# A sliding-window mix and an ELU MLP on one core: another prologue before the first token block

## The reference

```python
# x (4, 4096, 192), weight_gen (4, 4096, 8, 7), w_in (192, 2048), w_out (2048, 192), all float32
w = exp(weight_gen - max over the 7 taps);  w = w / (sum over the taps + 1e-9)
x_pad = x with 6 zero tokens in front of each sequence
mixed[b, s, h, :] = sum over k of w[b, s, h, k] * x_pad[b, s + k, h, :]     # 8 heads of 24 channels
h = mixed.reshape(16384, 192) @ w_in
g = where(h > 0, h, exp(min(h, 0)) - 1)
out = g @ w_out
```

## Time and profile before

| what | us |
|---|---|
| median of 3 runs (1242.32 to 1243.68) | 1242.58 |
| the profiled execution's own time | 1241.61 |
| its span | 1239.8 |
| TensorE busy | 1203.3 |
| ScalarE busy | 968.9 |
| VectorE busy | 822.3 |
| GpSimd busy | 705.1 |

### The profile page before, as it was taken

How to read it: one execution, slowest core, us unless ns; L and a number is a source line. 1 busy time by engine, 2 the same in 40 slices (tenths; PEclk the granted TensorE clock), 3 DMA queues, 4 the chain that set the end, 5 groups by cost and what they waited for, 6 DMA issues and landing times.

```text
span 1239.8 us, 19812 instructions
## 1 busy us (share of the span) xinstructions
PE 1203.3 (97%) x6848; PEld 1088.5 (88%) x6848; DVE 822.3 (66%) x1453; ACT 968.9 (78%) x1897; POOL 705.1 (57%) x298
## 2 busy tenths in 40 slices
PE   2699999999999999999999999999999999999998
PEld 1699999999999999999999999999999999999998
DVE  7866666666666666666666666666666666666665
ACT  3588787888788788787787787887887887888786
POOL 8677654567545576554576555576554676555600
PEclk9899999999999999999999999999999999999999
DMA  7011011111011110011110111110111110110000
GB/s 228 33 49 35 15 50 48 48 49 34 14 48 49 48 48 23 26 48 49 48 48 14 35 48 48 49 48 3 46 49 48 48 49 0 48 49 13 13 13 13
DMA packets 17086, 51.82 MB, mean 42 GB/s; under 512 B 1944, under 2 KB 8212, under 8 KB 17040
## 3 DMA queue, kind: packets, MB, share of 16 engines
q1 hardware_dynamic: 17040, 51.36, 12.5%
HBM read 38.77 MB, written 12.58 MB: 41 GB/s over the span
## 4 chain that ended last, share of the span: by engine, by line
PE 96%; DVE 3%; ACT 0%; DMA 0%; SPq 0%; POOL 0%; issue 0%; DVEq 0%; POOLq 0%
PE slot L599 48%; PE acc L605 29%; PE acc L609 17%; DVE wout L509 1%; PE slot L587 1%; PE slot L589 1%; DVE prod L477 0%; DVE prod L481 0%; DMA xwin<-in_x_dram 0%; SPq L248 0%; DVE prod L485 0%; DVE slot L554 0%; DVE g_lo L560 0%; DVE prod L487 0%; POOL xwin L293 0%
## 5 line engine op out<-in xcount | busy, mean ns | idle before, releaser
L554 DVE SCALAR_TENSOR_TENSOR slot<-em,slot 128x512 f32<-128x512 f32 x512 | 356.3, 696 | 388.2 <-ACT em L437 386.5
L605 PE MATMUL acc<-wout,g_hi 128*128 128x384 f32 x2048 | 468.2, 342 | 9.5 <-DVE g_lo L560 9.5
L431 ACT ACTIVATE em<-slot 128x512 f32<-128x512 f32 x512 | 305.0, 596 | 194.1 <-PE slot L599 194.1
L605 PEld LDWEIGHTS acc<-wout,g_hi 128*128 128x128 f32 x2048 | 369.2, 188 | 46.5 <-issue 9.9
L560 DVE TENSOR_TENSOR g_lo<-slot,g_hi 128x512 fp32r<-128x512 f32 x511 | 349.9, 685 | 1.9
L437 ACT ACTIVATE em<-em 128x512 f32<-128x512 f32 x512 | 323.5, 632 | 16.4
L609 PE MATMUL acc<-wout,g_lo 128*128 128x192 f32 x2048 | 326.7, 266 | 0.2 <-DVE g_lo L560 0.2
L609 PEld LDWEIGHTS acc<-wout,g_lo 128*128 128x128 f32 x2048 | 311.8, 190 | 3.0 <-DVE g_lo L560 0.5
L337 POOL TENSOR_TENSOR prod<-xwin,probs 128x5376 f32<-128x5376 f32 (+1 forms) x32 | 308.2, 9631 | 8.1 <-POOL probs L323 6.5
L444 ACT ACTIVATE g_hi<-slot 128x512 fp32r<-128x512 f32 x511 | 298.3, 584 | 13.1 <-DVE slot L554 11.6
L599 PE MATMUL slot<-xt,win_hi 128*128 128x512 f32 x512 | 214.6, 419 | 2.7 <-DVE xt L522 2.7
(11 more groups left out here) (47 smaller groups left out, 586.0 us busy)
## 6 DMA issues: line engine op xcount, KB each, us to landing
xwin<-in_x_dram SPq DMA_DIRECT2D x30, 960.0 KB, 4.8
out_dram<-outs SPq DMA_DIRECT2D x32, 384.0 KB, 2.4
wg<-in_weight_gen_dram SPq DMA_DIRECT2D x32, 112.0 KB, 2.3
wout_raw<-in_moe_w_out_dram SPq DMA_DIRECT2D x4, 384.0 KB, 9.0
win_raw<-in_moe_w_in_dram SPq DMA_DIRECT2D x1, 768.0 KB, 6.2
win_rest_raw<-in_moe_w_in_dram SPq DMA_DIRECT2D x2, 384.0 KB, 8.2
xwin<-in_x_dram SPq DMA_DIRECT2D x1, 768.0 KB, 10.5
xwin<-in_x_dram SPq DMA_DIRECT2D x1, 384.0 KB, 4.1
```

The costliest lines, as they stand in the source:

```text
L431: nc.scalar.activation(em[:, i % 2, :], slot[s][:], ACT.Exp).then_inc(s_exp, 1)
L554: nc.vector.scalar_tensor_tensor(out=slot[s][:], in0=em[:, i % 2, :], scalar=0.0, in1=slot[s][:], op0=ALU.min, op1=ALU.max).then_inc(s_g, 1)
L605: pe.matmul(acc[j][:, 0:2 * d_model], g_hi[:, f % GBUFS, chunk(j)], wout[:, f, :], start=(f == 0), stop=False)
```

## The change

- **Joint softmax.** The weights of blocks 0 and 1 are loaded first, and one softmax over both (64 rows of 7 per partition) runs on VectorE and ScalarE; GpSimd only scales.
- **The mix of block 0.** VectorE takes tiles 0 and 1 (before: 0 to 2). Its scaled weights go to a PSUM slot, the products of taps 0 to 3 to the four accumulator banks, those of taps 4 to 6 to SBUF, and each sum takes one input from PSUM. GpSimd takes tiles 2 and 3.
- **Part loads.** Four of the eight of window 0 are issued by ScalarE's queue.
- **Weights.** w_in comes in four quarters, like w_out. For the first two quarters of w_in and the first of w_out ScalarE writes the high half a second time, into PSUM (`mirror`), and VectorE's low half is the raw value in SBUF minus that copy. The low halves of all other quarters are GpSimd's: three after the products of block 1's mix, three after its pair sums, one after its last sums. Their high halves are ScalarE's, at chunks 0, 1, 2, 4, 5, 6 and 8 of block 0.
- **First chunks in halves.** Tiles 0 and 1 are transposed first, and the first three first products run over their 256 tokens; then the same for tiles 2 and 3.
- **Softmax of block 2** stands at chunks 5, 8, 9 and 12 of block 0 (7, 10, 11 and 12 before).

```diff
-            sp.dma_start(wg[:, 0, :], wg_v[:, 0:TILES, :]).then_inc(s_wg[0], 16)
+            for n in range(2):
+                sp.dma_start(wg[:, n, :], wg_v[:, n * TILES:(n + 1) * TILES, :]).then_inc(s_wg[n], 16)
             sp.dma_start(xwin[:, 0, halo:, :], x_v[:, 0:TILES, :]).then_inc(s_x[0], 16)
...
+            sp.wait_ge(s_zero, 1)
+            for at in range(0, P // 2, parts_per_batch):
+                reach_back(sp, 0, at)
...
+            load_win(0)
+            load_win(1)
+            load_wout(0)
             sp.dma_start(xwin[:, 1, halo - TILES:, :], x_v[:, 0:2 * TILES, :]).then_inc(s_x[1], 16)
+            sp.wait_ge(s_zero, 2)
+            for at in range(0, P, parts_per_batch):
+                reach_back(sp, 1, at)
+            load_wout(1)
+            load_win(2)
+            load_wout(2)
+            load_win(3)
+            load_wout(3)
...
@@ GpSimd, from block 1's mix on @@
+            pool.wait_ge(s_x[1], 16)
+            pool.wait_ge(s_reach[1], 16 * batch * len(REACH_PARTS))
+            pool.wait_ge(s_vmix, VMIX)
+            pool.wait_ge(s_add, ADDS)
+            products(1, 0, TILES // 2, last=False)
+            products(1, TILES // 2, TILES)
+            low_half("out", 1)
+            low_half("in", 2)
+            low_half("rest", 2)
+            pair_sums(one_)
+            shifted(two_)
+            low_half("out", 2)
+            low_half("in", 3)
+            low_half("rest", 3)
+            last_sums(one_)
+            guarded(two_)
+            low_half("out", 3)
...
@@ ScalarE @@
+            for kind, bank in (("in", slot[2][:]), ("rest", slot[3][:])):
+                hi_half(kind, 0)
+                mirror(kind, 0, bank)
+            hi_half("in", 1)
+            hi_half("rest", 1)
+            hi_of_pair(0, 0, 0, 1)
+            act.wait_ge(s_vmix, VMIX)
+            mirror("in", 1, acc[0])
+            mirror("rest", 1, acc[1])
+            hi_half("out", 0)
+            mirror("out", 0, wout_banks())
+            hi_of_pair(0, 1, 1, 2)
...
@@ VectorE, after its mix @@
+            low_half("in", 0, slot[2][:])
+            low_half("rest", 0, slot[3][:])
+            lo_of_pair(0, 0, 0, XPARTS)
+            low_half("in", 1, acc[0])
+            low_half("rest", 1, acc[1])
+            low_half("out", 0, wout_banks())
+            lo_of_pair(0, 1, 1, 2 * XPARTS)
...
@@ TensorE @@
             for k in range(X_STEPS):
-                if (k + 1) * PAIR > VECTOR_TILES:
+                if k == 1:
                     pe.wait_ge(s_add, ADDS)
                 transposes(0, k, k)
-            pe.wait_ge(s_wlo, 2)
-
-            pe.wait_ge(s_xlo, XPARTS * X_STEPS)
-            for f in range(LAG):
-                first_product(0, f, slot_of(0, f))
+                if k == 0:
+                    pe.wait_ge(s_wlo, 2)
+                pe.wait_ge(s_xhi, XPARTS * (k + 1))
+                for f in range(LAG):
+                    first_product(0, f, slot_of(0, f), slice(k * W, (k + 1) * W), filled=(k == 1),
+                                  when=XPARTS * (k + 1) if f == 0 else None)
```

More of the change, by code:

```diff
@@ L327, in body @@
[L327 to L338, removed]
+                r = slice(first_tile * heads, ROWS)
@@ new lines, in scaled, with products @@
+                nc.gpsimd.tensor_tensor(rows(probs[:, q, :])[:, r, :], rows(probs[:, q, :])[:, r, :],
+                                        spread(rec, kernel)[:, r, :], ALU.mult).then_inc(s_psoft, 1)
+            def products(q, first, end, last=True):
+                done = nc.gpsimd.tensor_tensor(prod_of(first, end), taps_of(q, first, end), weights_of(q, first, end),
+                                               ALU.mult)
+                if last:
+                    done.then_inc(s_prod, 1)
@@ L359, in softmax_vector @@
+            body(two_)
+            body(Block(1, 1))
+            with pool.Fori(2, BLOCKS // 2) as pair:
+                for parity in range(2):
+                    body(Block(pair, parity))
         def softmax_vector(b, step):
@@ new lines, in _, with spread @@
+            both_probs = probs[:].rearrange("p q (r k) -> p (q r) k", k=kernel)
+            def spread(t, k):
+                return t.unsqueeze(2).broadcast_to([P, t.shape[1], k])
+            for q in range(2):
+                dve.wait_ge(s_wg[q], 16)
+            nc.vector.tensor_reduce(first_max[:], both, AX.X, ALU.max).then_inc(s_vsoft, 2)
+            dve.wait_ge(s_vsoft, 2)
+            nc.vector.tensor_tensor(both_probs, both, spread(first_max[:], kernel), ALU.subtract).then_inc(s_psoft, 2)
@@ new lines, in _ @@
+            nc.vector.tensor_tensor(prod[:, BANK_TAPS:, 0:end].rearrange("p k (r g) -> p k r g", g=group),
+                                    taps_of(0, 0, VECTOR_TILES, (BANK_TAPS, kernel)), bank_weights((BANK_TAPS, kernel)),
+                                    ALU.mult).then_inc(s_vmix, 1)
+            dve.wait_ge(s_vmix, 3)
+            nc.vector.tensor_tensor(prod[:, BANK_TAPS:, 0:end], banks[:, 0:half, :], prod[:, BANK_TAPS:, 0:end],
+                                    ALU.add).then_inc(s_vmix, 1)
@@ new lines, in _ @@
+            total = banks[:, half, :]
+            for k in range(half - 1):
+                dve.wait_ge(s_vmix, 4 + k)
+                nc.vector.tensor_tensor(total, total, prod[:, BANK_TAPS + k, 0:end], ALU.add).then_inc(s_vmix, 1)
+            dve.wait_ge(s_vmix, 6)
+            total_t = total.rearrange("p (t d) -> p t d", d=d_model)
+            last_t = prod[:, kernel - 1, 0:end].rearrange("p (t d) -> p t d", d=d_model)
+            nc.vector.tensor_tensor(mixed[:, 0, 0:VECTOR_TILES, :], total_t[:, :, 0:P], last_t[:, :, 0:P],
+                                    ALU.add).then_inc(s_vmix, 1)
```

280 lines of the change are left out of this document (160 added, 120 removed).

## The result

The changed kernel takes **1231.61 us** (median of 4 runs, 1230.49 to 1233.91); the kernel before, run beside it, 1242.45 (1242.28 to 1243.68). The ratio is 0.991, 95% interval 0.9898 to 0.9923. The forecast was 1229.5 with a range of 1226 to 1235. The profiled execution is the fastest of the four: 1230.49 with a span of 1228.7, so its times are good for places and lengths, and 1.1 us too good for the total.

A forecast was written before the change was run, and what follows sets the result against it. Block 0's slow start, with VectorE and GpSimd taking turns, costs time beyond TensorE's pace. GpSimd's chain 48.95 + 18.04 = 67.0 against 80.10 gains 13.1; 1241.61 - 13.1 = 1228.5, plus 1.0 to the median: 1229.5 us, range 1226 to 1235.

The forecast's parts named there:

- Rival 1: Window loads come late because the two queues' issues take turns: 1.7 us more, 1231.2 us (1233 if worse); chance 0.14.
- Rival 2: TensorE's clock falls during its wait at block 1's transposes, costing 2.3 us: 1231.8 us; chance 0.16.
- The mark: The critical chain's entry when block 0 ends, 80.10 before; forecast at 67.0, a gain of 13.1 us.
- The start of the mixes: Block 0's prologue: joint softmax (3.4 us) done at 6.75, then GpSimd's scaling 0.35 and a turn of 0.25: 7.35.
- GpSimd's first tiles: GpSimd's mix of tiles 2 and 3 in block 0: 10.43 us plus 0.2 of fixed parts, ending at 18.0.
- Window 1: Block 1's token window, for which GpSimd would wait after its scaling, until 19.5 (bounds 17.5 and 21.6).
- Six low halves: GpSimd's low halves ahead of the last sums of block 1's mix: 3584 elements, 8.0 us.
- Transposes to mark: TensorE from the transposes of block 1's first two tiles to the end of block 0: 18.04 us.
- TensorE's own chain: Block 0: first exponential at 22.4, second products at 26.8, transposes reached at 45.3, 3.6 us ahead of GpSimd.
- one of the signs that the prediction named for being wrong: TensorE waiting elsewhere in block 0 (for g_lo or a weight), window 1 landing past 22, or block 1 waiting too.
- Rival 3: GpSimd isn't last in block 0; TensorE's chain ends it at 63.3, a gain of 16.8: 1225.8 us; chance 0.13.
- Rival 4: VectorE instructions with one PSUM input still keep GpSimd out: block 0 ends at 87.5, 1250 us; chance 0.03.

The follow-up runs named there:

- experiment 4: Two kernels: the change with all eight window 0 part loads on the sync queue, 1232.42 us; with early activation-table load and weights held until window 0 landed, 1232.28 us.
- window ahead of the weights: The changed kernel with the activation table loaded early and the loads of w_in and w_out held back until window 0 has landed: 1232.28 us.
- the early table: The changed kernel with a tiny exponential first on ScalarE to load the activation table, its tile allocated last so no other moves: 1229.62 us.
- all loads on sync: The changed kernel with all eight part loads of window 0 issued by the sync queue, as before the change: 1232.42 us.
- whole chunks: The changed kernel with block 0's first three chunks whole (512 tokens) after both pairs of tiles: 1231.92 us.
- the late copy: The changed kernel with ScalarE's copy of quarter 1 of w_out moved one chunk later: 1231.97 us.
- low halves from SBUF: The changed kernel without the PSUM copies; VectorE's five low halves of the prologue subtract the high half in SBUF: 1232.79 us.
- the sums first: The changed kernel with GpSimd's last sums of block 1's mix ahead of the second three low halves: 1229.02 us.
- both combinations: The changed kernel with activation table loaded early and last sums ahead of the second three low halves: 1228.56 us; also with w_out quarter 1's copy one chunk later: 1228.32 us.

## Why the prediction was right, and where it was off

The mechanism was right: turns between VectorE and GpSimd set the old start; with one PSUM input they end; GpSimd becomes the last, and TensorE meets it at block 1's transposes. The number is further off than the mechanism: 1231.61 lies inside the range, but 0.6 above the 1228 to 1231 that the prediction gave its own forecast, and nearer to the times of rivals 1 and 2. That it is the forecast's mechanism is known from the profile and the experiments, not from the time. The mark was forecast at 67.0 and came at 68.98, step by step:

- **The start of the mixes**, 7.35 forecast, 9.48 measured: +2.1, the one term that was mis-sized badly. The softmax was taken as 3.4 us of work between 2.68 and 5.36; it took 4.98 (3.62 to 8.60), because 1.28 of table load stands in it, a term that the sum put at nothing, and 0.3 more of work; it also began 0.3 later than the 3.33 of the sum. Before, that load ran at 0.74, under everything; now it stands behind the wait for VectorE's subtraction, and experiment 4 shows that this is not for the DMA issues in front of it. (The ScalarE: Activation LUTs page of the Trainium skill, "What ACT_TABLE_LOAD costs", has about 1283 ns for the load; the trace agrees.) And the window, forecast at 6.1 from its 2.46 in the earlier trace rows, landed at 9.31: a transfer's old duration was carried over although the loads behind it had been moved up against it (some 1.5 of the 3.2 us), and although the DMA engines were busy with loads ahead of it (the rest, as argued in experiment 4). Table and window cost about the same place twice: taking the load away won 0.6, not 1.2.
- **GpSimd's first tiles**, 10.65 forecast, 10.91 measured: +0.3. VectorE's mix took 6.54 with its scaling, the wait of 0.52 left out (6.5 forecast).
- **Window 1**: forecast to be waited for until 19.5; it never was, the scaling just took its 0.6: -0.9.
- **Block 1's products**, 9.8: 9.80.
- **Six low halves**, 8.0: 4.29 + 4.30 = 8.6, +0.6. They ran at 2.40 to 2.62 ns an element, where 2.14 to 2.25 was taken from longer ones.
- **Sums and shift**, 11.66: 11.4, -0.2.
- **Transposes to mark**, 18.04: 18.11, +0.1.

Together +2.0; the median lies 1.1 above the profiled execution, where 1.0 was assumed. TensorE's own chain was off by more: forecast at the transposes at 45.3, there at 49.9. 2.1 of it is the late start, 0.7 more had arisen by the first exponential (25.21 for 22.4) and 0.2 by the second products (29.82 for 26.8); the other 1.6 fell in the chunks behind them, where the clock was low and ScalarE had copies to make besides; how it divides between the two was not measured. It did not count, since GpSimd was later still, but it is why the wait was 0.97 and not 3.6. Its 2.28 us of waiting for `g_lo` at 29.82 is one of the signs that the prediction named for being wrong; the end in the profiled execution didn't depend on it, since TensorE waited for GpSimd afterwards.

Two rows were misread in the prediction. The 2.68 us of the old softmax run to the start of GpSimd's scaling (5.56); the reciprocal ends at 5.48, after 2.60. And the five matmuls of 2.49 in the earlier trace rows stand in a stretch (24.8 to 27.3) whose granted clock is shown at full; where it is shown at 0.50, five take 2.19 (window ahead of the weights, from 55.43). The first moves the sum by under 0.1; the second stands in rival 2 only, whose 2.3 us don't use it.

**Rival 1** (loads late, 1231.2) comes close to the time, by another mechanism: the queues didn't take turns, window 0 was late because it shared the DMA engines with other loads, and window 1 was not waited for. **Rival 2** (clock falls in the wait, 1231.8) did not happen in the profiled execution at the place it names, but does so in others: seven of the twelve kernels of the experiments had the lower clock behind that wait. Its price is read there: from the transposes to the mark it is 18.11 in the change and with the early table, and 19.68, 19.67 and 19.67 with all loads on sync, whole chunks and the late copy, so 1.56 us. With the low halves from SBUF it is 19.57 and with the 8-byte tile 19.76 (18.15 with that tile and no fall), and with the window ahead of the weights, where the clock fell while TensorE still waited, 20.52. So it is **1.5 to 1.6 us** in most and 2.4 in one, where 2.3 was estimated. That the change's other three runs, 1.1 to 3.4 above the profiled one, have this drop is likely but was only argued: no trace of them exists. **Rival 3** (GpSimd not last) is refuted by the chain and by the sums first. **Rival 4** (turns stay) is refuted by the undisturbed products and by VectorE's 0.70 at most from the first exponential on.

## What to carry to other kernels

Before giving a shared engine's work to the neighbour, add up the neighbour's chain to the next thing that waits for it: here that chain decided the gain, and the order of its pieces was worth another 2.6 us. When issues are moved up in a queue, price the transfers anew, since what was behind a transfer is now beside it. And when the start of ScalarE's program changes, look in the new trace where its table load went: here it moved from under everything into the chain, and the obvious cause was not the cause.

## What was not expected of the hardware

- An unused tile of 8 bytes per partition ahead of the steady state's tiles made each block of 37.42 us one of 37.57, for 31 blocks (two kernels, both with it; the one with the same edit and nothing moved had 37.42). Which of the moved tiles minds, and whether 16 bytes would do, was not tried.
- TensorE's clock was at its lower level behind waits of 2.24, 2.31, 2.36, 2.44, 2.96, 3.49 and 3.84 us at the transposes, and at full behind 0.97, 2.38 and 2.52: the length of the wait alone didn't tell.
- The runs of kernels in which TensorE does not wait at the transposes lie within 0.8 us (sums first, and both combinations); those of the change and the other kernels made from it spread over 1.3 to 3.9.
